# Attention and two expert layers on one core: value and gate products widened to 128 streamed columns

## What is computed

```python
def _attn_ref(q, k, v, n_global, n_local):          # B, H, S, D = 4, 8, 768, 64
    scores = scale * np.matmul(q, k.transpose(0, 1, 3, 2))
    ...
    keep = is_global | is_local                     # 8 global keys, 96 local ones
    scores = scores + bias[None, :, :, :]
    scores = np.where(keep, scores, -1000000000.0)
    scores = scores - np.max(scores, axis=-1, keepdims=True)
    a = np.exp(scores)
    a = a / (np.sum(a, axis=-1, keepdims=True) + 1e-09)
    return np.matmul(a, v)
...
x = attn_out.transpose(0, 2, 1, 3).reshape(B * S, H * D)
# first expert layer: skip_score = x @ w_skip; logits = x @ w_gate; top expert of 8, relu(x w1) w2
# second expert layer: logits = x @ w_gate; every expert takes N // 8 tokens
```

## Time and profile before

| | us |
|---|---|
| median of two runs | 1123.74 (1120.84 to 1126.64) |
| profiled execution, its own time | 1127.58 |
| its span, first to last instruction | 1125.8 |
| PE busy | 854.9 (76%) |
| DVE busy | 588.8 (52%) |
| ACT busy | 445.5 (40%) |
| mean granted TensorE clock | 0.812 |

### The profile page before, as it was taken

The page is one execution under the profiler, slowest core; times in us unless marked ns, Lnnn a source line. Parts: engine busy times, 40 slices in busy tenths (PEclk is TensorE's granted clock), DMA queues, the critical chain, the costliest instruction groups (busy, mean ns, idle before and its releaser), DMA issues. The chain is left out here.

```text
span 1125.8 us, 18804 instructions
## 1 busy us (share of the span) xinstructions
PE 854.9 (76%) x5391; PEld 784.1 (70%) x5391; DVE 588.8 (52%) x1424; ACT 445.5 (40%) x1015; POOL 153.7 (14%) x219
## 2 busy tenths in 40 slices
PE   0688988989985389999999611111269999999995
PEld 0588988889885379999999510111258999889994
DVE  4564463752752466566666136656635644556541
ACT  0676675963861054455555100000023433334420
POOL 1000010010000112223222200000020222112211
PEclk9877777965965579999999855555559999999998
DMA  4977689669503445564543040000034435455310
GB/s 74 200 170 159 193 170 259 133 150 254 114 9 118 159 151 202 193 223 172 181 173 101 15 153 1 0 0 0 0 127 154 148 126 193 177 177 171 124 68 28
DMA packets 106512, 146.89 MB, mean 130 GB/s; under 512 B 35558, under 2 KB 63462, under 8 KB 106480
## 3 DMA queue, kind: packets, MB, share of 16 engines
q1 hardware_dynamic: 92848, 114.96, 36.8%
q0 software_dynamic: 7360, 18.96, 5.2%
q10 hardware_dynamic: 6272, 12.58, 3.0%
HBM read 125.86 MB, written 23.76 MB: 133 GB/s over the span
## 5 line engine op out<-in xcount | busy, mean ns | idle before, releaser
L359 PE MATMUL m_ph<-m_xh,m_w1h 128*128 128x256 f32 (+1 forms) x544 | 170.8, 314 | 1.3 <-issue 1.3
L359 PE MATMUL m_ph<-m_xh,m_w1l 128*128 128x256 f32 (+1 forms) x544 | 168.3, 309 | 0.0
L359 PE MATMUL m_ph<-m_xl,m_w1h 128*128 128x256 f32 (+1 forms) x544 | 168.3, 309 | 0.0
L419 ACT ACTIVATE m_hh<-m_ph 128x256 fp32r<-128x256 f32 (+1 forms) x136 | 59.2, 435 | 255.7 <-PE m_ph L359 248.6
L406 ACT ACTIVATE m_w1h<-m_w 128x1024 fp32r<-128x1024 f32 x68 | 68.1, 1054 | 216.7 <-ACTq L64 187.0
L373 PE MATMUL m_py<-m_w2h,m_hh 128*128 128x512 f32 x336 | 135.2, 402 | 0.0
L373 PE MATMUL m_py<-m_w2l,m_hh 128*128 128x512 f32 x336 | 132.7, 395 | 0.0
L373 PE MATMUL m_py<-m_w2h,m_hl 128*128 128x512 f32 x336 | 132.7, 395 | 0.0
L462 DVE SCALAR_TENSOR_TENSOR m_hl<-m_ph,m_hh 128x256 fp32r<-128x256 f32 (+1 forms) x136 | 66.2, 487 | 110.7 <-ACT m_hh L419 107.1
L359 PEld LDWEIGHTS m_ph<-m_xh,m_w1h 128*128 128x128 f32 x544 | 104.0, 191 | 3.1 <-issue 2.4
L359 PEld LDWEIGHTS m_ph<-m_xl,m_w1h 128*128 128x128 f32 x544 | 104.0, 191 | 0.7
(11 more groups left out here) (203 smaller groups left out, 1474.5 us busy)
## 6 DMA issues: line engine op xcount, KB each, us to landing
m_w<-moe_w SPq DMA_DIRECT2D x34, 2048.0 KB, 9.2
q_raw<-qT SPq DMA_DIRECT2D x32, 384.0 KB, 5.8
x_rows<-xb ACTq DMA_DIRECT2D x8, 1536.0 KB, 9.5
k_raw<-kT SPq DMA_DIRECT2D x64, 160.0 KB, 4.5
k_raw<-kT SPq DMA_DIRECT2D x64, 120.0 KB, 4.6
vo<-vL SPq DMA_DIRECT2D x16, 384.0 KB, 3.3
vp<-vL SPq DMA_DIRECT2D x16, 240.0 KB, 4.3
k_raw<-kT SPq DMA_DIRECT2D x32, 64.0 KB, 4.4
```

Source lines behind the costliest of these rows:

```text
L359: last = nc.tensor.matmul(ph[m % 4][:, 0:tokens], w[:, c, m * P:(m + 1) * P], x[s][:, c, :], start=(c == 0 and a == 0), stop=(c == KC - 1 ...
```

## The change

The value products stream 128 columns of `vo` or `vp` in place of 64, that is the tile's own 64 and the 64 that stand behind them in the buffer, and write 128 columns of `op`; the second half falls on the next tile's columns, which that tile's first product (start=True) overwrites, or behind the last tile's. For this the two buffers become flat with 64 more columns at the end, which DVE sets to zero. The gate products stream 128 columns of a flat `wg1` from the same start on and write 128 columns of `lp` in place of 17; the next tile's products overwrite the rest. `wg1` has 128 more columns, set to zero by POOL in the set-up. The order of instructions on each engine is the same but for these memsets (one on POOL, four on DVE). The path for other mask sizes (`general`) has new slices and is not run.

```diff
-        wg1 = sb("wg1", [P, KC, G1])
+        wg1 = sb("wg1", [P, KC * G1 + P])
+        wg1_cols = wg1[:, 0:KC * G1].rearrange("p (c e) -> p c e", e=G1)
...
+                link(g.memset(wg1[:, KC * G1:], 0.0))
...
-                        last = nc.tensor.matmul(lp[:, (i - 1) * 32:(i - 1) * 32 + width], xs[(i - 1) % 2][:, c * P:(c + 1) * P],
-                                                wg[:, c, :], start=(c == 0), stop=(c == KC - 1))
+                        last = nc.tensor.matmul(lp[:, (i - 1) * 32:(i - 1) * 32 + P], xs[(i - 1) % 2][:, c * P:(c + 1) * P],
+                                                wg[:, c * width:c * width + P], start=(c == 0), stop=(c == KC - 1))
...
-            vo = [tb(f"vo{s}", [P, 2, QT_N, D]) for s in range(2)]
-            vp = [tb(f"vp{s}", [CA, 2, QT_N - 1, D]) for s in range(2)]
+            vo = [tb(f"vo{s}", [P, (2 * QT_N + 1) * D]) for s in range(2)]
+            vp = [tb(f"vp{s}", [CA, (2 * (QT_N - 1) + 1) * D]) for s in range(2)]
...
+            def v_own(s, hh, i):
+                return vo[s][:, (QT_N * hh + i) * D:(QT_N * hh + i + 2) * D]
+
+            def v_band(s, hh, i):
+                return vp[s][:, ((QT_N - 1) * hh + i) * D:((QT_N - 1) * hh + i + 2) * D]
...
-                        o = op[hd % 2][:, i * D:(i + 1) * D]
-                        last = nc.tensor.matmul(o, w[:, t * P:(t + 1) * P], vo[s][:, hh, i, :], start=True, stop=(i == 0))
+                        o = op[hd % 2][:, i * D:(i + 2) * D]
+                        last = nc.tensor.matmul(o, w[:, t * P:(t + 1) * P], v_own(s, hh, i), start=True, stop=(i == 0))
                         if i:
                             c = 2 if t else 3
-                            last = nc.tensor.matmul(o, w[0:CA, c * P:(c + 1) * P], vp[s][:, hh, i - 1, :],
+                            last = nc.tensor.matmul(o, w[0:CA, c * P:(c + 1) * P], v_band(s, hh, i - 1),
                                                     start=False, stop=True)
...
+                        v.memset(vo[s][:, 2 * QT_N * D:], 0.0).then_inc(biased, 1)
+                        v.memset(vp[s][:, 2 * (QT_N - 1) * D:], 0.0).then_inc(biased, 1)
```

More of the change, by code:

```diff
@@ L548, in _ @@
                 sp.dma_start(ints[:, 1:2], n_local.partition_broadcast(P)).then_inc(loaded, 16)
-                sp.dma_start(wg1[:, :, 0:E + 1], w_gate1.rearrange("(c p) e -> p c e", p=P)).then_inc(loaded, 16)
+                sp.dma_start(wg1_cols[:, :, 0:E + 1], w_gate1.rearrange("(c p) e -> p c e", p=P)).then_inc(loaded, 16)
                 sp.dma_start(wg2[:], w_gate2.rearrange("(c p) e -> p c e", p=P)).then_inc(loaded, 16)
-                sp.dma_start(wg1[:, :, E + 1:], w_gate2.rearrange("(c p) e -> p c e", p=P)).then_inc(loaded, 16)
+                sp.dma_start(wg1_cols[:, :, E + 1:], w_gate2.rearrange("(c p) e -> p c e", p=P)).then_inc(loaded, 16)
                 sp.dma_start(flip_t[:], flips.partition_broadcast(P)).then_inc(loaded, 16)
@@ L763, in fast @@
                             at(sp, summed[s], 6 * use)
-                            sp.dma_start(vo[s][:].rearrange("p h i d -> p (h i d)"), v2).then_inc(loaded[s], 16)
-                            sp.dma_start(vp[s][FAST_GLOBAL:CA].rearrange("p h i d -> p h (i d)"),
+                            sp.dma_start(vo[s][:, 0:2 * QT_N * D], v2).then_inc(loaded[s], 16)
+                            sp.dma_start(vp[s][FAST_GLOBAL:CA, 0:2 * (QT_N - 1) * D].rearrange("p (h m) -> p h m", h=2),
                                          v2[P - FAST_LOCAL:P].rearrange("p (h m) -> p h m", h=2)[:, :, 0:(QT_N - 1) * D]
@@ L774, in general @@
                         sp.dma_start(kd[:], k2).then_inc(d_loaded, 16)
-                        sp.dma_start(vo[0][:].rearrange("p h i d -> p (h i d)"), v2).then_inc(d_loaded, 16)
+                        sp.dma_start(vo[0][:, 0:2 * QT_N * D], v2).then_inc(d_loaded, 16)
                 by_path(sp, fast, general)
@@ L794, in fast @@
                             for hh in range(2):
-                                nc.gpsimd.tensor_copy(vp[s][0:FAST_GLOBAL, hh],
-                                                      vo[s][0:FAST_GLOBAL, hh, 0:1, :].broadcast_to([FAST_GLOBAL, QT_N - 1, D])
+                                nc.gpsimd.tensor_copy(vp[s][0:FAST_GLOBAL, (QT_N - 1) * D * hh:(QT_N - 1) * D * (hh + 1)].rearrange("p (i d) -> p i d", d=D),
+                                                      vo[s][0:FAST_GLOBAL, QT_N * D * hh:QT_N * D * hh + D].unsqueeze(1).broadcast_to([FAST_GLOBAL, QT_N - 1, D])
                                                       ).then_inc(fixed[s], 1)
@@ L886, in turn @@
                     for c in range(QT_N):
-                        last = nc.tensor.matmul(op[0][:, 0:D], prt[c // 4][:, (c % 4) * P:(c % 4 + 1) * P], vo[0][:, hh, c, :],
+                        last = nc.tensor.matmul(op[0][:, 0:D], prt[c // 4][:, (c % 4) * P:(c % 4 + 1) * P], vo[0][:, (QT_N * hh + c) * D:(QT_N * hh + c + 1) * D],
                                                 start=(c == 0), stop=(c == QT_N - 1))
@@ L1024, in fast @@
                         v.memset(kk[s][:, :, KW:].bitcast(F32), 0.0).then_inc(biased, 1)
-                    dve.wait_ge(biased, 2 * H + 4)
+                        v.memset(vo[s][:, 2 * QT_N * D:], 0.0).then_inc(biased, 1)
+                        v.memset(vp[s][:, 2 * (QT_N - 1) * D:], 0.0).then_inc(biased, 1)
+                    dve.wait_ge(biased, 2 * H + 8)
                     for c in range(PARTS):
```

## The result

The changed kernel takes 1081.76 us (median of two runs, 1080.30 and 1083.22) against 1123.74 before: ratio 0.963, 95% interval 0.951 to 0.975. The forecast was 1081. A second measurement on one chip gave 1082.65 (four runs, 1080.69 to 1083.79), with the kernel before at 1121.56 (13 runs), ratio 0.967 (0.960 to 0.975). Medians and ranges hold all runs; each ratio leaves out those more than 1.5% above the fastest run of their kernel. The spread is a result too: the kernel before ran from 1111.7 to 1138.2 us, the changed one within 3.1 us.

A forecast was written before the change was run, and what follows sets the result against it. PE at half clock, 160.6 us of the attention stage, was taken to set the pace there. Gate stages 18 plus pairs and batch starts 26.4 minus wider passes 2 made 42.4 us, from 1123.74 to 1081 us, range 1062 to 1103.

The forecast's parts named there:

- The clock answers to the width of the passes: Attention's PE passes: few columns do less to keep or regain full clock; half-level time from 161 us to under 40.
- A wider pass costs nothing up to 128 columns: Value and gate passes: spacing stays 112 ns at full and 213 ns at half clock; lower bound of added time zero.
- The term of 2 us: Cost of widening 704 value and 192 gate records, 2 ns a pass on average, subtracted from the gain.
- The estimated slope of 0.13 ns a column: Alternative cost of wider passes: 8 ns for 64 more columns, some 8 us over 896 passes.
- Gate stages: Four gate stages stay at full clock, about 9.5 us each, saving 3.6 + 3.7 + 5.8 + 4.9 = 18 us.
- Pairs behind a load stall: Head pair after ACT's wait for k and q: 17.2 us becomes 14.2, 3 us in each of four batches, 12 us.
- Starts of batches: Batches 2 to 4 start at half clock with slow score passes: 1.5 us saved each, 4.5 in sum.
- What is late next: k and q load of each batch's third pair: 2 us of room; if crowded, each batch loses one or two us.
- ACT the busiest engine of the stage: Sign of being right: in the attention stage ACT becomes the busiest engine; no size given.
- The rival that only the gate stages gain: Padded values do not shorten half spells after stalls: 18 of 44 us, about 1106; chance 0.13 including part of the values.
- The third rival: Stream and weight load add up and the clock stays: up to 91 us more, near 1210; chance of slower 0.04.

The follow-up runs named there:

- the layout alone: Changed kernel's flat buffers and memsets, but value products of 64 and gate products of 17 columns as before: 1123.5 us, ratio 1.003 to the kernel before.
- each part alone: Against the kernel before: only value products 128 columns wide, 1099.59 us, ratio 0.984; only gate products 128 wide, 1105.15 us, ratio 0.987.
- the gate-only kernel: Changed kernel with gate products 128 columns wide but value products of 64 as before: 1105.15 us, ratio 0.987 to the kernel before.

## Why the prediction was right

The time came out within 1 us, and the mechanism by its own steps:

- *The clock answers to the width of the passes.* Shown: the layout alone saves nothing, each part alone saves about its share, and with both wide no half spell in attention is longer than 6.8 us. What was not shown is when a fall comes: two executions of the same changed kernel differ in it.
- *A wider pass costs nothing up to 128 columns.* Shown: 0.22 us a pair at full clock and 0.42 at half, as with 64 columns; 256 columns cost 217 ns a pass. The term of 2 us was too large: per tile of the gate stage, passes and transposes together take 1.33 us in place of 1.29 (102.00 to 103.33 and, with 17 columns, 101.25 to 102.54), 1 us over the four stages, and a unit's eight value passes with the step to what follows take 0.90 us (median) at either width. The estimated slope of 0.13 ns a column, worked out from the two figures of the Trainium skill (TensorE: Matmul & The Clock Gate, "Back-to-back issue gap"), would be 14 ns a pass from 17 to 128 columns; the median distance does not grow at all.
- *Gate stages.* Forecast 9.5 us each and 18 us in sum. They take 9.25 (98.94 to 108.19 in the first), and with the lengths before of 13.0, 13.2, 15.3 and 14.4 us the four save 19.
- *Pairs behind a load stall.* Forecast 3 us each. The one of the earlier trace rows saves 4.7 (17.2 to 12.4), the three others 3.9 to 5.1. I had added 0.7 us for refilling and 1.0 for the half spell; neither shows, since ACT is busy for the whole spell and hides it. This term was some 7 us too small.
- *Starts of batches.* Forecast 1.5 us each. From the first scores to the first pair's end it was 16.65 us (120.53 to 137.18) and is 16.11 (108.19 to 124.30), a saving of 0.5. The first passes run faster, but they were no longer the bound after a few us. This term was 3 us too large.
- *What is late next.* I looked at the third pair of a batch and gave it 2 us of room; no wait appeared there. The waits that did appear are in the second and fourth pair of the first batch, where the loads had not been late before: ACT waits 0.55 and 1.48 us for k until 57.23 and 86.20, and the two pairs take 1.1 and 1.7 us longer than before. (The third pair's wait, until 72.08, is the old one of 3.72 us, now 2.20.) I had not looked there.
- *ACT the busiest engine of the stage.* This sign did not come: PE has matmuls in flight for 224.8 of 269.0 us and ACT is busy for 207.6.

The misses cancel in part: the terms sum to 42.4, and the attention stages of the two traces differ by 48. I also subtracted the gain from a profiled execution that took 1127.6 us, near the upper part of that kernel's own spread; with 1120 to 1123 us as its usual time the median gain is 39 to 42 us and not the 47 of the two traces. The forecast passed through 42.4, a number that was too small for the pair of traces and fitted the medians by luck.

The rival that only the gate stages gain would have been 1106 us, and the gate-only kernel took 1105: its price was right, and its condition, that padded values do nothing, false. The third rival's price of 91 us gives 1215 and not 1210; nothing hangs on it.

## What to carry to other kernels

If the granted clock sits at half level while TensorE's records follow each other without a gap, look at how many columns a pass streams. Here, where each f32 pass comes with its own weight load, up to 128 columns a pass cost next to nothing, and 64 or 111 more useless columns a pass bought 3.3 to 3.7% of the whole program. Measure the spacing before you pad: at 256 columns it had doubled. Pad as far as is free in every stage, since one stage of narrow passes loses the level for the next; then look for the pauses that are left, and remove those last, because without the width that gave less than 1%.

## What the runs showed of the hardware that I had not expected

- Half of the added width is not enough in the gate stage, though it sometimes does: 64-column gate passes left the clock at half for 17 to 24 us in four stages and had it back after 6.8 in one, where 128-column ones had it back within 10.2 us at most (behind 96-column values), which includes the value passes ahead of them.
- Pauses of about 1 us can stand ahead of a fall at either width: 0.7 and 1.1 us among 64-column values (51 us at half behind it), 1.13 and 0.91 us among 128-column ones (3.4 us at half). The changed kernel, with pauses of 0.80 and 0.98 us at the start of its gate stages, kept the full level in all four of them in both profiled executions. So a pause of that length does not decide it alone.
- The spread between executions shrank from 26.5 us (13 runs) to 3.1 us (4 runs). Over those 13 runs of the kernel before, the mean granted clock goes from 0.834 in the fastest (1111.66 us) to 0.803 in the slowest (1138.2 us), and almost every longer run has the lower clock, so the spread goes with the clock. At which places the falls moved was seen in the profiled executions alone.
